# Sums of probabilities from a column of ones beside the values, both tails of a pair added in one block, the output copied by ACT, biases made on chip

## What is computed

```python
# attention: batch 4, heads 8, seq 576, head_dim 64
scores = q @ k.T / 8
mask = (rel >= 0) & (rel < 128)                    # rel = query position - key position
scores = where(mask, scores - slope[h] * abs(rel), -1e9)
attn = exp(scores - max(scores))
attn = attn / (sum(attn) + 1e-09)
x = attn @ v                                       # then [4 * 576 tokens, 512]
h = x @ w_in;  g = h / (1 + exp(-1.702 * h));  x = g @ w_out      # d_ff 2048
h = x @ w_in2; g = where(h >= 1, h, where(h <= -1, 0, (h + 1) ** 2 / 4)); out = g @ w_out2
```

## Time and profile before

| | us |
| --- | --- |
| median of 3 runs | 900.24 |
| lowest and highest | 898.88, 900.36 |
| the profiled execution | 900.17 |
| its span, first to last instruction | 898.4 |
| mean granted TensorE clock, share of full | 0.98 |

### The profile page before, as it was taken

One profiled execution on the slowest core, in us unless ns is written; L12 is line 12 of the kernel. 1 busy time (PEld: TensorE's weight loads), 2 busy tenths in 40 slices (PEclk: granted clock), 3 DMA queues, 4 the chain that ended last, 5 costly groups with the idle time before them and its releaser, 6 DMA issues.

```text
span 898.4 us, 15742 instructions
## 1 busy us (share of the span) xinstructions
PE 863.4 (96%) x5730; PEld 854.8 (95%) x5730; DVE 733.8 (82%) x1035; ACT 543.5 (60%) x918; POOL 107.7 (12%) x75
## 2 busy tenths in 40 slices
PE   5988888889999999999999999999999999999998
PEld 5988888889999999999999999999999999999998
DVE  5788899676779886777898987888989779889794
ACT  3668767656677553676764445766655467765431
POOL 2677678200000000000000000000000000000000
PEclk7899999999999999999999999999999999999999
DMA  9986866055856635758676466188763662879822
GB/s 215 243 218 156 227 186 185 28 196 208 309 205 223 246 132 209 258 226 309 248 247 249 173 235 246 71 314 299 236 212 132 229 243 98 289 274 317 291 92 71
DMA packets 64075, 191.93 MB, mean 214 GB/s; under 512 B 7552, under 2 KB 15104, under 8 KB 60160
## 3 DMA queue, kind: packets, MB, share of 16 engines
q1 hardware_dynamic: 64000, 190.93, 63.2%
HBM read 118.55 MB, written 72.35 MB: 212 GB/s over the span
## 4 chain that ended last, share of the span: by engine, by line
PE 87%; DVE 6%; issue 5%; ACT 1%; SPq 1%; DMA 0%; DVEq 0%; ACTq 0%
PE ps L950 77%; PE ps L883 3%; PE ps L918 3%; PE ps L896 2%; DVE qk_hi L1400 1%; DVE probs L1430 1%; PE ps L911 1%; DVE k_lo L1403 1%; DMA bias_sb<-bias_table 0%; DVE wst L1469 0%; DVE x_pairs L1451 0%; DVE probs_tail L1430 0%; DVE w_first L1476 0%; PE ps L927 0%; PE ps L932 0%
## 5 line engine op out<-in xcount | busy, mean ns | idle before, releaser
L950 PE MATMUL ps<-arena,w_first 128*128 128x384 f32 x1764 | 332.2, 337 | 2.6 <-ACT ps L1199 1.2
L950 PEld LDWEIGHTS ps<-arena,w_first 128*128 128x128 f32 x1764 | 310.7, 188 | 4.8 <-issue 3.4
L950 PE MATMUL ps<-arena,w_rest 128*128 128x384 f32 x1260 | 240.8, 337 | 0.9 <-ACT ps L1179 0.8
L950 PEld LDWEIGHTS ps<-arena,w_rest 128*128 128x128 f32 x1260 | 220.1, 188 | 2.0 <-issue 1.7
L1525 DVE TENSOR_TENSOR arena<-raw_first,arena 128x768 fp32r<-128x768 f32 (+1 forms) x116 | 150.8, 1313 | 78.2 <-ACT arena L1153 78.2
L1153 ACT ACTIVATE arena<-raw_first 128x768 fp32r<-128x768 f32 (+1 forms) x120 | 131.8, 1117 | 48.7 <-DVE raw_first L1510 39.7
L950 PE MATMUL ps<-w_rest,arena 128*128 128x256 f32 x945 | 132.4, 281 | 0.0
L950 PEld LDWEIGHTS ps<-w_rest,arena 128*128 128x128 f32 x945 | 121.1, 189 | 0.1
L950 PE MATMUL ps<-w_first,arena 128*128 128x256 f32 x567 | 88.0, 282 | 0.0
L1525 DVE TENSOR_TENSOR arena<-raw_rest,arena 128x1536 fp32r<-128x1536 f32 (+1 forms) x48 | 71.4, 1487 | 12.0 <-ACT arena L1153 11.9
L950 PEld LDWEIGHTS ps<-w_first,arena 128*128 128x128 f32 x567 | 76.0, 189 | 0.0
(11 more groups left out here) (110 smaller groups left out, 1030.5 us busy)
## 6 DMA issues: line engine op xcount, KB each, us to landing
gd<-g SPq DMA_DIRECT2D x24, 1536.0 KB, 6.1
raw_rest<-gd SPq DMA_DIRECT2D x32, 768.0 KB, 5.0
qk_raw<-qkT SPq DMA_DIRECT2D x62, 288.0 KB, 5.5
wst<-w_pairs SPq DMA_DIRECT2D x32, 512.0 KB, 6.1
raw_first<-gd SPq DMA_DIRECT2D x16, 768.0 KB, 5.9
yd<-ust SPq DMA_DIRECT2D x6, 1536.0 KB, 6.3
wd<-ust SPq DMA_DIRECT2D x4, 1536.0 KB, 9.1
raw_first<-yd SPq DMA_DIRECT2D x4, 1536.0 KB, 7.0
```

Source lines behind the costliest of these rows:

```text
L950: last = nc.tensor.matmul(to, stationary, moving, start=start and n == 0, stop=n == len(steps) - 1, skip_group_check=True)
```

## The change

- **Values.** Beside the 64 columns of v stands one of ones (`VALUES` = 65), supplied by the host. Weighing the values gives the sum of probabilities as column 64. The ten outputs of a pair (8 blocks, 2 tails) lie in two banks, five to a bank, 65 columns each (`o_banks`). `sums`, the accumulation in ACT's exponentials and `guard_sums` are gone. DVE adds 1e-9 to the ten sums in PSUM, inverts them, and writes all 640 columns of `heads_out` by one operation.
- **Tails.** Odd heads are stored in another order (queries' tail, queries, keys), with 64 columns of zeros before or behind, so that the tail queries of the even head fill rows 0 to 63 and those of the odd head rows 64 to 127. Both are added up in one block of 256 columns, and DVE biases them by one operation with 128 rows. PE's instructions in this step are as many as before.
- **Output copy.** `copy_pair` moves from DVE to ACT, at the same lag; the tail's copy stays on DVE.
- **Biases.** One table of distances (128x448) is loaded instead of 8 tables of 128x256. ACT multiplies it by the slopes (`make_bias`, three operations a pair), for pair 0 first of all, for pairs 1 to 3 behind the exponentials of steps 1, 6 and 11.
- **Splits.** `DVE_HEADS` shrinks from seven heads to 0, 1 and 3; the other splits go to POOL. The odd head's CAST stands 3 steps behind the pair's end instead of 1 (`ODD_LAG`).
- **Start.** PE starts its dummy matmuls as soon as the arena is cleared, does 16 more behind the first scores (`KEEP_WARM`), and waits for the identity only then.
- **Seam.** `mark_written` of banks 5 and 6 moves ahead of `product_6` and no longer waits for the last tail copy; the next duo does. ACT copies the last pair behind its first two seeds.

```diff
-DVE_HEADS = (0, 1, 13, 19, 25, 29, 31)
+DVE_HEADS = (0, 1, 3)
+KEEP_WARM = 16
+ODD_LAG = 3
...
-        sp.dma_start(bias_sb[:, 0], bias_table[:, 0]).then_inc(bias_in[0], 16)
+        sp.dma_start(distance[:], bias_table).then_inc(distance_in, 16)
...
         for h in range(1, HEADS):
             load_operands(h)
-            sp.dma_start(bias_sb[:, h], bias_table[:, h]).then_inc(bias_in[h], 16)
             load_values(h - 1)
...
         def scores(m):
...
+                query0 = QUERIES_AT[e] + blk * P if blk < 4 else TAIL_AT[e]
+                queries = qk_hi[:, head % SPLIT_RING, query0:query0 + P]
+                place = bank[:, i * BAND:(i + 1) * BAND] if d else bank[:, 0:BAND]
+                for n_pass, k in enumerate((keys(qk_hi, head), k_lo[:, head % SPLIT_RING])):
+                    last = nc.tensor.matmul(place, queries, k[:, key0:key0 + BAND],
+                                            start=n_pass == 0 and (d > 0 or i == 0), stop=n_pass == 1 and (d > 0 or i == 1))
...
-                    last = nc.tensor.matmul(o_bank[:, at:at + DIM], probs_t[:, gi % 2, col:col + P],
+                    last = nc.tensor.matmul(o_slot(2 * blk + e), probs_t[:, gi % 2, col:col + P],
                                             v_sb[:, h + e, max(blk - 1, 0) + piece],
...
                 transpose_pair(PAIR_COUNT - 1)
+                mark_written(5)
+                mark_written(6)
                 product_6(u, up, c, k, D, 0)
                 product_5(u, up, c, k, D, 1)
                 transpose_pair_tail(PAIR_COUNT - 1)
-                pe.wait_ge(pair_tail_copied, PAIR_COUNT)
-                mark_written(5)
-                mark_written(6)
                 product_6(u, up, c, k, D, 1)
...
-        pe.wait_ge(cleared, 5)
-        warm_up()
-        pe.wait_ge(ident_in, 16)
+        pe.wait_ge(cleared, 1)
+        warm_up(WARM_UP)
         for m in range(ALL_STEPS + VALUE_LAG):
             if m < ALL_STEPS:
                 scores(m)
+            if m == 0:
+                warm_up(KEEP_WARM)
+                pe.wait_ge(ident_in, 16)
...
-                last = nc.scalar.activation(at, at, ACT.Exp, bias=neg_max[:, col:col + 1], scale=-1.0,
-                                            accum_out=sums[:, q % SUM_RING, 2 * blk + e:2 * blk + e + 1])
+                last = nc.scalar.activation(at, at, ACT.Exp, bias=neg_max[:, col:col + 1], scale=-1.0)
...
-        def guard_sums(q):
...
+        def make_bias(pair):
+
+            act.wait_ge(distance_in, 16)
+            for h in (2 * pair, 2 * pair + 1):
+                nc.scalar.activation(bias_sb[:, h], distance[:, 0:BAND], ACT.Copy, scale=SLOPES[h]).then_inc(bias_made, 1)
+            nc.scalar.activation(bias_tail[:, pair], distance[:, BAND:BAND + TAIL_KEYS], ACT.Copy,
+                                 scale=SLOPES[2 * pair]).then_inc(bias_made, 1)
+
+        def copy_pair(q):
+            pair = q % BATCH_PAIRS
+            act.wait_ge(pair_transposed, q + 1)
+            wait_past(act, x_stored[pair], 16 * (q // BATCH_PAIRS))
+            nc.scalar.activation(x_pairs[:, pair, 0:4 * P], xt_bank, ACT.Copy).then_inc(pair_copied, 1)
...
+            dve.sem_inc(dve_gate, 1)
+            if d == 0:
+                to, col = probs_tail[:, q % TAIL_RING, 0:TAIL_KEYS], 2 * (STEPS - 1) + q % TAIL_RING
+                last = nc.vector.tensor_tensor_reduce(out=to, in0=bank[:, TAIL:BAND], in1=bias_tail[:, q % BATCH_PAIRS],
...
         def write_pair(q):
-            s = q % SUM_RING
+            at = inverse[:, q % SUM_RING]
+            dve.wait_ge(pv_done, 4 * (q + 1))
+            nc.vector.tensor_scalar(at, o_banks[:, :, :, DIM], 1e-9, None, ALU.add).then_inc(sums_guarded, 1)
             dve.wait_ge(sums_guarded, q + 1)
-            nc.vector.reciprocal(inverse[:, s], inverse[:, s]).then_inc(sums_inverted, 1)
+            nc.vector.reciprocal(at, at).then_inc(sums_inverted, 1)
             dve.wait_ge(sums_inverted, q + 1)
-            dve.wait_ge(pv_done, 4 * (q + 1))
...
-            nc.vector.tensor_tensor(heads_tail[:, q % 2], tail_bank[:, 0:P],
-                                    inverse[:, s, 8:9].to_broadcast([P, P]), ALU.mult).then_inc(pair_written, 1)
+            nc.vector.tensor_tensor(heads_out[:, q % 2].rearrange("p (b s d) -> p b s d", b=2, d=DIM), o_banks[:, :, :, 0:DIM],
+                                    at.unsqueeze(3).to_broadcast([P, 2, SLOTS // 2, DIM]), ALU.mult).then_inc(pair_written, 1)
...
-            if (q := pair_at(m, 1)) is not None and q + 2 < PAIR_COUNT:
+            if (q := pair_at(m, ODD_LAG)) is not None and q + 2 < PAIR_COUNT:
                 round_head(2 * q + 5)
-            if (q := pair_at(m, COPY_LAG)) is not None:
-                copy_pair(q)
```

More of the change, by code:

```diff
@@ L54 @@
 FIRST_COLS = 3 * P
[L55 removed]
+DVE_HEADS = (0, 1, 3)
 WARM_UP = 22
+KEEP_WARM = 16
+WIDTH = 2 * SEQ + TAIL
+KEYS_AT = (0, TAIL + SEQ)
+QUERIES_AT = (SEQ, 2 * TAIL)
+TAIL_AT = (SEQ + 4 * P, 0)
+ZEROS_AT = (2 * SEQ, 0)
+LOADED_AT = (0, TAIL)
+VALUES = DIM + 1
+SLOTS = 10
 TRANSPOSE_LAG = 2
@@ L66 @@
 X_STORE_LAG = 6
+ODD_LAG = 3
+CLEARED = 6
+SLOPES = tuple(2.0 ** (-8.0 * (h + 1) / HEADS) for h in range(HEADS))
 HALF = 384
@@ L143, in build @@
     pt_bank = [ps[:, i] for i in (3, 7)]
-    tail_bank = ps[:, 2]
-    o_bank = ps[:, 5]
-    xt_bank = ps[:, 6]
+    xt_bank = ps[:, 2]
+    o_banks = ps[:, 5:7, 0:SLOTS // 2 * VALUES].rearrange("p b (s n) -> p b s n", n=VALUES)
     ident_in = sem("ident_in")
-    bias_in = [sem(f"bias_in{i}") for i in range(HEADS)]
+    distance_in = sem("distance_in")
+    bias_made = sem("bias_made")
     qk_in = [sem(f"qk_in{i}") for i in range(SPLIT_RING)]
@@ L499, in load_operands @@
             for half in range(2):
-                sp.dma_start(qk_raw[half * DIM:(half + 1) * DIM, slot], qkT[head]).then_inc(qk_in[slot], 16)
+                sp.dma_start(loaded(qk_raw, head)[half * DIM:(half + 1) * DIM], qkT[head]).then_inc(qk_in[slot], 16)
         def load_values(head):
@@ L858, in _, with warm_up @@
     def _(pe):
-        def warm_up():
-            for _ in range(WARM_UP):
-                nc.tensor.matmul(o_bank[:, 0:BAND], arena[:, 0:P], arena[:, P:P + BAND], start=True, stop=True)
+        def warm_up(count):
+            for _ in range(count):
+                nc.tensor.matmul(ps[:, 5, 0:BAND], arena[:, 0:P], arena[:, P:P + BAND], start=True, stop=True)
         def scores(m):
@@ L875, in scores @@
             bank = score_bank[m % SCORE_RING]
-            for i, (e, blk) in enumerate(ITEMS[d] or ((0, 4), (1, 4))):
-                slot = (2 * q + e) % SPLIT_RING
+            items = ITEMS[d] or ((0, 4), (1, 4))
+            for i, (e, blk) in enumerate(items):
+                head = 2 * q + e
                 key0 = max(blk - 1, 0) * P if blk < 4 else SEQ - BAND
[L880 to L884, removed]
+                query0 = QUERIES_AT[e] + blk * P if blk < 4 else TAIL_AT[e]
[4 more added lines that the diff above has]
+                                            start=n_pass == 0 and (d > 0 or i == 0), stop=n_pass == 1 and (d > 0 or i == 1))
             last.then_inc(scores_ready, 1)
@@ L1374, in _ @@
         nc.vector.memset(v_sb[TAIL:P, :, 4], 0.0).then_inc(cleared, 1)
-        nc.vector.memset(sums[:], 1.0).then_inc(cleared, 1)
+        for e in range(2):
+            nc.vector.memset(f32(qk_hi[:, e::2, ZEROS_AT[e]:ZEROS_AT[e] + TAIL]), 0.0).then_inc(cleared, 1)
         nc.vector.memset(half[:], 0.5).then_inc(cleared, 1)
@@ L1411, in bias_scores @@
             bank = score_bank[m % SCORE_RING]
-            if q < BATCH_PAIRS and d in (2, 3, 0):
-                for e in range(2):
-                    dve.wait_ge(bias_in[h + e], 16)
+            if q == 0:
+                dve.wait_ge(bias_made, (3, 3, 1, 2, 2)[d])
+            elif q < BATCH_PAIRS and d == 0:
+                dve.wait_ge(bias_made, 3 * q + 3)
             dve.wait_ge(scores_ready, m + 1)
@@ L1767, in bias_constants @@
     row = np.arange(P)[:, None]
-    col = np.arange(BAND)[None, :]
-    rel = P + row - col
-    slopes = 2.0 ** (-8.0 * (np.arange(HEADS, dtype=np.float32) + 1) / HEADS)
-    bias = -slopes[:, None, None] * np.abs(rel)[None].astype(np.float32)
-    table = np.where((rel >= 0) & (rel < WINDOW), bias, -1e9) / SCALE
-    return np.ascontiguousarray(table.transpose(1, 0, 2).astype(np.float32))
+    rel = P + row - np.arange(BAND)[None, :]
+    table = np.where((rel >= 0) & (rel < WINDOW), -np.abs(rel), -1e9 * 2.0 ** HEADS) / SCALE
+    tails = np.concatenate([table[0:TAIL, 0:TAIL_KEYS], table[TAIL:P, TAIL:BAND] / 2])
+    return np.concatenate([table, tails], axis=1).astype(np.float32)
 def kernel(q, k, v, moe_w_in, moe_w_out, moe2_w_in, moe2_w_out):
```

122 lines of the change are left out of this document (61 added, 61 removed).

## The result

The changed kernel took **910.65 us** (median of 4, 909.35 to 911.94), the kernel before 900.17 (median of 4): ratio 1.012, 95% interval 1.010 to 1.014. It is 1.2% slower, where 894.4 was forecast and 902 was the upper end of the range. The profiled execution took 911.26, its span is 909.4.

What follows compares the result with a forecast made beforehand. The attention stage was taken as bound by a loop of dependences, at least 9.5 us a round (PE 8.1, wait 1.4). Gains of 2.6 (rounds), 2.1 (start) and 1.1 (end), 5.8 off 900.17, gave 894.4; range 887 to 902.

Steps and rivals of the forecast that it cites:

- The start: Before pair 1: step 0 starts near 20.0 us instead of 23.28; 1.2 given back next round, net gain 2.1.
- The chain from step 2: Odd head's biases, CAST and two POOL subtractions, 5.5 us from step 2's scores to the next pair's step 0.
- the 1.4: New PE wait before step 0 in every round: 5.5 us of chain against 4.1 of PE work.
- its two falls: PE's clock falls behind two of the five waits of 2.0 us, costing 1.2 each, 2.4 us.
- the gap of 1.74: PE gap before 90.11 us in the kernel before; clock stayed 1.00, so waits of 1.4 should do nothing.
- POOL's weight and operand steps: On POOL, up to 1.83 us each; behind both heads in five rounds, adding 0.6, so 10.1 each.
- End: Around pair 15: the long wait before it and the half clock behind it go; net gain 1.1 us.
- DVE's relief: DVE in the attention stage falls from 8.3 busy us a round to some 6.5 and stops being a limit.
- ACT's copy: Moved output copy, ahead of PE's tail transposition: hidden while ACT keeps pace; if not, a few tenths a round.
- 65 columns: PE's value matmuls, 64 to 65 columns: between nothing and 10 us, taken as nothing; rival at +10, about 904, chance 0.02.
- The slower end: Rival: PE's regular wait before step 0 pulls the clock down in nearly every round; 914 us, chance 0.10.
- the four: Rivals: no clock fall, 888 (0.22); new wait replaces old, 897 to 901 (0.18); clock, 914 (0.10); 65 columns, 904 (0.02).

Runs made afterwards that it cites:

- the first experiment: The changed kernel with one edit: POOL splits operand S2 behind head 31 instead of behind head 30; 901.99 us.
- third experiments: The changed kernel with ODD_LAG 1, S2's split behind head 31 and S1's split behind head 29 instead of 28; 891.47 us.
- the fourth experiment: The changed kernel with ODD_LAG 1, both splits moved (S1 behind head 29, S2 behind 31) and the 512-column output copy back on DVE; 886.70 us.
- The seventh: The kernel before with only DVE_HEADS cut to 0, 1 and 3, and S1 and S2 split behind heads 29 and 31; 888.15 us.

## Why the prediction was wrong

**The start held.** Step 0 of pair 1 starts at 19.84 (predicted 20.0), head 1's CAST at 9.73. Pair 2 starts at 31.55, where the sum had 30.7: 0.9 too early. That is partly this execution's clock: it is 0.50 from 21 to 24 us, and 1.00 in the profile of the first experiment, which has the same code up to there and its pair 2 at 29.13.

**The chain from step 2 held, to a tenth.** Predicted 5.5 us from the first scores of step 2 to those of step 0. In the changed kernel, PE, DVE and POOL in order of time, answering to the earlier trace rows:

```profile
54.92 0.37 PE L920 MATMUL ps<-qk_hi 128*128 128x256 f32 x1
56.57 0.75 DVE L1449 CAST qk_hi<-qk_raw 128x1152 fp32r<-128x1152 f32 x1
57.47 1.41 POOL L824 TENSOR_TENSOR k_lo<-qk_raw,qk_hi 128x576 fp32r<-128x576 f32 x1 [0.76 <-DVE qk_hi L1449]
58.95 1.40 POOL L827 TENSOR_TENSOR qk_hi<-qk_raw,qk_hi 64x576 fp32r<-64x576 f32 x1
60.46 0.36 PE L920 MATMUL ps<-qk_hi 128*128 128x256 f32 x1 [0.76 <-issue]
```

54.92 to 60.46 is 5.54. Of the 1.4 the profile shows 0.76 as PE's idle time before step 0 and 0.2 on the way, for ACT's copy; the rest isn't shown as a wait, and part of it at least lies under modelled ends of matmuls. The 11 rounds from pair 2 to pair 13 took 110.1 us; the sum with its two falls gives 109.3 for them. That close a total is in part luck. Five rounds are 9.5, where the sum had nine; three others that it put at 9.5 took 9.9, 10.5 and 11.1, and the clock fell once there, behind the wait of 2.39 before pair 11, not twice. (The clock at 87 to 90, taken as that behind the gap of 1.74, is that of the gap itself, which ends at 90.11; from 90 to 96 it was 1.00 too, so the conclusion stands.)

**The step that failed: POOL's other work had a length but no wait.** The prediction priced POOL's weight and operand steps at up to 1.83 each, put the rounds before pairs 14 and 15 at 10.1 and 9.5, and said under **End** that the long wait before pair 15 goes. They took 12.1 and 19.5, and that wait, 2.8 us for DVE's copy before, became 8.04 for POOL. It had asked what POOL's steps delay by their length. It didn't ask what they wait for. S1's and S2's splits wait for ACT's roundings behind steps 66 and 74, and an in-order queue passes such a wait on to all that stands behind it. The rows to read were among the waits of the kernel before, and on its POOL in order of time:

```profile
POOL arena L828 <- ACT arena L1153: 14.3, 3, 8.9
...
167.39 1.83 POOL L828 TENSOR_TENSOR arena<-raw_first,arena 128x768 fp32r<-128x768 f32 x1 [8.87 <-ACT arena L1153]
```

Three waits of POOL for ACT's arena, 14.3 us in all. The longest is that of S2's split, behind head 30, and it did no harm, since head 31 was on DVE. The change put head 31 behind it. The rounds from pair 13 to pair 15 took 31.6 us where the sum had 19.6: **12.0 of the 16.9 us** between the forecast and the profiled execution (911.26). The first and third experiments put 8.7 on S2's place and 3.2 on S1's. For S2 it is the wait; for S1 the greater part is the split's own length, 1.83, which the prediction did have, against a wait of 1.30 in the changed kernel.

**The end** was put at 1.1 gained; behind the start of pair 15 the profile has 736.1 us against 734.1 before, so it is 3.0 off. Half clock behind the long wait is in it: with S2 moved, and the clock at 1.00 there, the same part takes 734.6. PE's wait for the write chain of the last pair is 0.85, where a like one was 0.7 before, so the longer chain costs little. What makes the rest isn't settled. The stretches show the clock behind the waits before pairs 14 and 15 (changed kernel, columns as in the earlier trace rows):

```profile
153.00:156.00 3.00, 2.17 (x11) 2.21 (x11) 0.36 (x2) 0.00 (x0) 2.84 (x3) 0.50 0.00 0
...
174.00:177.00 3.00, 3.00 (x18) 3.00 (x18) 0.37 (x2) 0.05 (x1) 0.00 (x0) 0.55 0.00 0
```

**The terms that nobody could see in the total.** DVE's relief was right in size: 91.9 of 160 us is 6.3 a round of 10.96, where 6.5 was forecast. Its worth was misread: DVE's total mattered less than where the splits of heads 13 to 31 stood. When the fourth experiment gave DVE the copy back, its busy time rose from 108.2 to 125.0 of the same 160 us, and the kernel became 4.8 us faster. The seventh gives 11 of the 12.5 us that lie between the kernel before and the fastest to moving the splits, with the order mended. ACT's copy was to be hidden or cost "a few tenths a round", and nothing went into the sum for it; it cost 4.8 over the stage, 0.34 a round. 65 columns cost nothing: 277 ns in the mean against 280.

**The rivals.** The slower end was put down to the clock, with a chance of 0.10. The clock does follow the long waits (0.50 in 153 to 156 us, behind the wait of 3.41), but between pairs 2 and 13 it fell once, and the regular wait of 0.75 left it at 1.00. The case that came wasn't among the four.

## What to carry to other kernels

Before work is moved onto an in-order queue, list for each instruction that then stands ahead of it what that one waits for, and not only how long it takes; a wait that costs nothing today is paid by whatever is queued behind it tomorrow. Here an engine with 53 of 160 us free idled 9.9 us, 5.6 of them in front of ready work, and one line of order was worth 8.7 us. Splitting a bundled change also pays: two of its edits (a lag and a copy) cost 7 and 5 us, one was worth 11 once the queue's order was mended, and all the rest about 1.5 together.

## What the runs showed of the hardware

A subtraction on DVE with two operands in SBUF took 0.76 us alone and 1.85 to 2.25 beside POOL's subtractions, and the CAST 0.76 and up to 2.42 (at 141.69 in the changed kernel): the price of a DVE instruction here depends on what POOL does at that moment by a factor of 2.4 to 3.2, more than was reckoned from the mean of 1.25. And executions of one kernel differ in the clock: the ten with S2 moved and lag 3 lie between 898.98 us at 0.994 and 905.67 at 0.982, the four with lag 1 within 0.6 at 0.992. That the lag is the cause isn't shown: other kernels with lag 1 scattered over 2.9 and 3.3 us, and the kernel before with lag 3 over 1.9. Why only some executions lose the clock isn't settled.
